# A one-core kernel in which each expert's TensorE program is set to a fixed place of its instruction blocks, with repeated waits left out

## What is computed

```python
def _moe2_ref(x, w_gate, w1, w2, capacity):      # 1536 tokens of 384, 8 experts, hidden 1024
    logits = x @ w_gate
    expert_idx = np.argmax(logits, axis=1)
    ...
    disp[e, counts[e]] = x[i]                    # each token into a row of its expert, at most 384 rows
    ...
    h = np.maximum(np.einsum('ecd,edf->ecf', disp, w1), 0.0)
    y = np.einsum('ecf,efd->ecd', h, w2)
    out[i] = gate_w[i] * y[expert_idx[i], pos[i]]
```

## Time and profile before

| | |
|---|---|
| runs: median, lowest, highest | 443.18, 442.60, 444.14 us |
| the profiled execution | 441.74 us, of which its span is 440.0 us |
| TensorE, matmuls | 413.5 us busy, 94% of the span |
| VectorE, ScalarE, GpSimd | 252.3, 192.7, 227.1 us busy |
| granted TensorE clock | 0.986 of full, mean of the span |

### The profile page before, as it was taken

How to read it: one execution, slowest core, us unless ns; L and a number is a source line. 1 busy time by engine, 2 the same in 40 slices (tenths; PEclk the granted TensorE clock), 3 DMA queues, 4 the chain that set the end, 5 groups by cost and what they waited for, 6 DMA issues and landing times.

```text
span 440.0 us, 9260 instructions
## 1 busy us (share of the span) xinstructions
PE 413.5 (94%) x3247; PEld 395.4 (90%) x3247; DVE 252.3 (57%) x515; ACT 192.7 (44%) x442; POOL 227.1 (52%) x237
## 2 busy tenths in 40 slices
PE   6799999999999999999999996889999999999783
PEld 5688889999999999999999995789999999998672
DVE  6888866766435434453347665353286696627840
ACT  2789944341311113111233332151668777437830
POOL 4999716554323533244365671521738476337942
PEclk9999999999999999999999999799999999999997
DMA  7996034536970100000003351285385786818300
GB/s 248 403 361 198 3 114 132 165 95 209 354 292 1 54 1 0 0 18 36 0 0 101 96 179 37 93 288 182 109 288 149 236 250 193 265 40 256 105 28 11
DMA packets 33938, 61.48 MB, mean 140 GB/s; under 512 B 4654, under 2 KB 26910, under 8 KB 33888
## 3 DMA queue, kind: packets, MB, share of 16 engines
q1 hardware_dynamic: 31008, 55.53, 38.4%
q0 software_dynamic: 2880, 5.29, 3.5%
HBM read 47.53 MB, written 14.79 MB: 142 GB/s over the span
## 4 chain that ended last, share of the span: by engine, by line
PE 79%; DVE 7%; ACT 5%; issue 4%; POOL 2%; DMA 0%; POOLq 0%; ACTq 0%; DVEq 0%
PE bank L1245 20%; PE bank L1260 20%; PE bank L1429 15%; PE bank L1393 10%; PE bank L1453 4%; ACT scores L632 3%; PE bank L1146 2%; PE bank L1360 1%; PE bank L1212 1%; ACT w_high L615 1%; DVE scores L879 1%; DVE neg L937 1%; PE bank L1176 1%; DVE act_full L943 1%; PE bank L1204 1%
## 5 line engine op out<-in xcount | busy, mean ns | idle before, releaser
L522 POOL TENSOR_TENSOR g_low<-act_full,g_high 128x384 fp32r<-128x384 f32 x63 | 63.6, 1010 | 114.6 <-ACT g_high L661 114.6
L661 ACT ACTIVATE g_high<-act_full 128x384 fp32r<-128x384 f32 x64 | 33.6, 526 | 149.9 <-DVE act_full L943 137.2
L1245 PE MATMUL bank<-x_split,w_high 128*128 (+1 forms) x384 | 98.4, 337 | 0.0
L937 DVE TENSOR_SCALAR neg<-bank,alpha_sb 128x384 f32<-128x384 f32 x64 | 39.2, 613 | 71.5 <-PE bank L1245 71.4
L589 POOL TENSOR_TENSOR w_low<-w_raw,w_high 128x384 fp32r<-128x384 f32 x48 | 50.0, 1074 | 46.9 <-ACT w_high L723 46.9
L1245 PEld LDWEIGHTS bank<-x_split,w_high 128*128 128x128 f32 x384 | 69.0, 188 | 0.2 <-issue 0.2
L1260 PE MATMUL bank<-w_high,g_high 128*128 128x384 f32 x189 | 65.1, 344 | 1.1 <-POOL g_low L522 1.1
L1245 PE MATMUL bank<-x_split,w_low 128*128 (+1 forms) x192 | 64.4, 336 | 0.0
L1260 PE MATMUL bank<-w_high,g_low 128*128 128x384 f32 x189 | 63.8, 337 | 0.0
L1260 PE MATMUL bank<-w_low,g_high 128*128 128x384 f32 x189 | 63.8, 337 | 0.0
L856 DVE TENSOR_TENSOR w_low<-w_raw,w_high 128x384 fp32r<-128x384 f32 x44 | 30.1, 689 | 28.5 <-ACT w_high L615 22.9
(11 more groups left out here) (138 smaller groups left out, 821.8 us busy)
## 6 DMA issues: line engine op xcount, KB each, us to landing
w_raw<-chunks SPq DMA_DIRECT2D x96, 192.0 KB, 4.5
w_raw<-chunks SPq DMA_DIRECT2D x32, 384.0 KB, 3.1
rk_in<-att_rk SPq DMA_DIRECT2D x12, 704.0 KB, 6.3
routed_rows<-fill SPq DMA_DIRECT2D x1, 5211.0 KB, 17.4
xe<-routed_rows SPq DMA_DIRECT2D x7, 579.0 KB
v_in<-att_v SPq DMA_DIRECT2D x12, 200.0 KB, 6.1
out<-fill SPq DMA_DIRECT2D x1, 2304.0 KB, 23.5
x_split<-x_split POOLq DMA_DIRECT2D x18, 48.0 KB, 2.5
```

The costliest lines, as they stand in the source:

```text
L522: pool.tensor_tensor(gl[:, f % 4, :], act_full[:, f % 2, :], gh[:, f % 4, :].bitcast(f32), ALU.subtract).then_inc(s_gl, 1)
L661: act.activation(gh[:, f % 4, :], act_full[:, f % 2, :], ACT.Copy).then_inc(s_gh, 1)
L937: dve.tensor_scalar(neg[:, f % 2, :], h, 0.0, alpha_sb[:, f:f + 1], ALU.min, ALU.mult)\
L1245: last = mm(bank[f % 4][:, 0:G], a[:, f, w], x[:, kc, bass.ds(g * G, G)], start=kc == 0 and i == 0, stop=kc == KC - 1 and i == 2)
```

## The change

It does two things to TensorE's program of the last stage, and nothing to the other engines.

Waits are left out where an equal or stronger one stands just before on the same engine. From expert 1 on, w_in's low parts are waited for at f = 0 and f = 4, four chunks at a time, not at each f; w_out's low parts once for all eight, at f = 0. The rows of experts 2 to 7 are waited for at their first tile alone, and the bank for tile 1's transposes with that for tile 0's. This makes experts 1 to 6 510 places long: 1, 78, 220, 1, 54 and 156.

```diff
@@ -52,6 +52,8 @@
     WARM = 3
     START_WARM = 22
     LEVELS = 7
+    FETCH = 256
+    INTO = 20
     RK = 4
     RH = 4
     assert P == 1 << LEVELS
@@ -1355,7 +1357,8 @@
                 if e == 1 and i == 0:
                     pe.wait_ge(s_tel, GT)
 
-                xe_there(pe, e, (i,))
+                if e < 2 or i == 0:
+                    xe_there(pe, e, (i,))
                 for kc in range(KC):
                     last = pe.transpose(dst[:, kc * P:(kc + 1) * P], xe[:, e % 2, i, kc * P:(kc + 1) * P], ident[:, :])
                 last.then_inc(s_te, 1)
@@ -1369,9 +1372,9 @@
 
             def x_bank_free(e, i):
 
-                if i < 2:
+                if i == 0:
                     y_bank_free(e, GT - 1 - i)
-                else:
+                elif i == 2:
                     pe.wait_ge(s_tel, e * GT + GT)
 
             def y_bank_free(e, i):
@@ -1381,7 +1384,10 @@
             def expert_up(e, f, n):
                 s = e * NFE + f
                 slot = s % SLOTS
-                w1_ready(pe, e, f)
+                if not e:
+                    w1_ready(pe, e, f)
+                elif f % HF == 0:
+                    w1_ready(pe, e, f + HF - 1)
                 if s >= 4:
 
                     pe.wait_ge(s_mgl, s - 3 + C_MGL)
@@ -1424,7 +1430,10 @@
                         pe.wait_ge(s_fl, 2 * e + f // HF + 1)
                     else:
                         pe.wait_ge(s_mgl, s + 1 + C_MGL)
-                    pe.wait_ge(s_wl2, s + NF + 1)
+                    if not e:
+                        pe.wait_ge(s_wl2, s + NF + 1)
+                    elif not f:
+                        pe.wait_ge(s_wl2, e * NFE + NFE + NF)
                     for m, (a, w) in enumerate(((egh, wh), (egh, wl), (egl, wh))):
                         last = mm(bank[4 + i][:, 0:DM], a[:, f, i * P:(i + 1) * P], w[:, s % SLOTS, W1:CW],
                                   start=f == 0 and m == 0, stop=f == NFE - 1 and m == 2)
@@ -1484,6 +1493,9 @@
                 turn_xe(0, i, bank[4 + i])
 
             for e in range(E):
+                if e:
+
+                    pe.addr_align(FETCH, offset=FETCH - INTO, max_nops=4)
                 with pe.If(rows[e] < P + 1):
                     pe.wait_ge(s_tel, e * GT + GT - 1)
                     pe.sem_inc(s_mh, NFE)
```

## The result

The changed kernel is slower: 447.18 us (445.14 to 449.64, 12 runs) against 442.87 us (441.95 to 444.14, 12 runs) of the kernel before beside it, a ratio of 1.0098 (95% interval 1.0078 to 1.0119). The forecast was 441.4 us with a range to 445.2. The profiled execution took 448.58 us, for a span of 446.8 us against 440.0. The twelve runs lie in two groups, six from 445.14 to 446.56 us and six from 447.79 to 449.64; the profiled one is of the upper group, so its 6.75 us more of span are more than the 4.31 us between the medians.

What follows compares the result with a forecast made beforehand. TensorE, busy 94% of the span, was taken to bound the kernel, with three instruction-fetch gaps near the end. Gains of 0.21 + 1.28 + 0.26 = 1.75 us, waits and padding 0, gave 443.18 - 1.75 = 441.4 us, range 439.8 to 445.2.

Steps and rivals of the forecast that it cites:

- What bounds the kernel: TensorE fills 94% of the span; three pieces of "issue" in the last three experts are instruction blocks arriving.
- The three gaps: TensorE pauses of 1.48, 1.28 and 0.26 us in the last three experts' tiles, read as waits for instructions.
- (a): Fixed places put each short branch's tile inside one block, removing its gaps: 0.21 + 1.28 + 0.26 = 1.75 us gained.
- second and third gaps: Pauses in the last two experts' tiles, claimed worth all of their 1.28 and 0.26 us.
- The first gap: Pause of 1.48 us in the third last expert's tile, claimed worth 0.21 us because VectorE's chain follows.
- cap in the scatters: Last scatter could start at 432.60; its forerunner at 431.06 allows 432.34, so scatters were taken not to limit the gain.
- The stated range: Range of 8 in 10 for the time, from 439.8 (3.02 plus 0.2 of the waits) to 445.2 us.
- both stretches are longer, if the packet starts promptly: Short experts have 4.9 and 6.2 us before needing the next block, against 2.3 to 2.8 us for its arrival.
- first rival: Blocks come late in a new place: three TensorE stands of 1.4 us at short experts' jumps, 445.0 us, chance 0.20.
- lies inside one block: The short branch's tile, offset 300 to 353, crosses no block boundary, so the three pauses cannot stay where they are.
- (c): Padding before experts, including some 220 dead places jumped before expert 1: 0 taken, bounds 0 to 1.5 us lost.
- (b): Leaving out repeated waits on TensorE: 0 taken, bounds 0 to 0.2 us gained.

Runs made afterwards that it cites:

- INTO = 120: Changed kernel with each expert from 1 on starting 120 places ahead of a block boundary, not 20: 440.61 us, ratio 0.9963; in more rounds 440.55 us, 0.996.
- added jump: Changed kernel plus one taken jump over one dead place, right behind the boundary at place 20, short branch only: 440.59 us, ratio 0.9967.
- control: Changed kernel plus the same dead place in the short branch, walked through as a filler instruction instead of jumped over: 447.15 us, ratio 1.0109.
- the last experiment: Kernel before with all its waits and one fixed place at expert 5, so experts 5 to 7 enter every block by a jump: 440.7 us, ratio 0.9965.

## Why the prediction was wrong, step by step

**What bounds the kernel: right.** The three gaps were the arrival of blocks, on the grid I had counted. The kernels with boundaries at 120, or with experts 5 to 7 moved, lose the second and the third. The other 27 of the 30 blocks before cost nothing that TensorE's chain shows. Expert 6's jump waited for its block: the branch of 415.77 lasts 3.37 us, where the taken ones of the kernel before last 0.21 to 0.37 us. The added jump and its control show that a jump can also set when the next block is asked for (packet at 410.76 with it, 416.61 without).

**(a), the worth of the gaps: right in size, where the blocks come in time.** TensorE's last matmul ends at 431.16 us with INTO = 120, against 432.86: 1.70 us earlier, forecast 1.75. That it comes so near is in part luck. Counted from expert 0's third tile (298.66 against 298.37) it is 1.99 us: 1.54 for the second and third gaps, nothing for the first, where I had 0.21, and most of the rest because a tile without a gap inside runs quicker (24 matmuls in 4.43 us in expert 7, 2.15 + 2.57 = 4.72 before). The first gap is worth next to nothing: INTO = 120 still has it (1.38 us), the added jump's kernel has not, and expert 6's tile starts at 416.07 and 416.88 in them, which is the same when counted from expert 0's third tile (298.66 and 299.48). Of the 1.70 us, though, only 1.23 reach the end. I had found no cap in the scatters; there is one, since the first of the last three waits for earlier ones to land. In the chain, and then the timeline of GpSimd, with INTO = 120:

```profile
425.11 4.27 DMA out<-y_out,token
...
425.11 0.97 POOL L580 DMA_INDIRECT out<-y_out,token  x1 [0.30 <-issue]
430.57 0.97 POOL L580 DMA_INDIRECT out<-y_out,token  x1 [4.49 <-issue]
431.84 0.97 POOL L580 DMA_INDIRECT out<-y_out,token  x1 [0.30 <-issue]
433.12 0.97 POOL L580 DMA_INDIRECT out<-y_out,token  x1 [0.30 <-issue]
```

The last starts at 433.12, not at the forecast 432.60, against 434.35 in the earlier trace rows; its forerunner, which I had left at 431.06, moved to 431.84.

The stated range has a slip that decides nothing: 443.18 less 3.02 and 0.2 is 439.96 us, not 439.8.

**The step that failed: "both stretches are longer, if the packet starts promptly".** I had 4.9 us from the boundary at 20 to the tile, against 2.3 to 2.8 us for a block, and took the request as made when the boundary is crossed. In expert 6 it was made only at the jump (415.77, packet 416.77), 4.17 us ahead of the first matmul. A row that warned of it stood in the prediction: the earlier trace rows, a packet 3.2 to 4.2 us late "with no other reason in sight". I gave it to the first rival with a chance of 0.20, and priced it there as a delay of that length, three times: 4.2 us less what is hidden. In fact expert 5 had no stand (its packet came 1.5 us after it walked in), expert 6 one of 3.67 us, expert 7 one of 1.08. The trace of before held, and I did not read, that all six packets of its last three experts start behind a taken jump; if only a jump asks, the 4.9 us are not there, and the stand is the whole of a fetch.

**That the branch's tile "lies inside one block": wrong for expert 7.** It has some 40 places fewer than the others (44 in the program before, less the left-out waits that stood among its missing transposes), which puts the start of its tile at about 260, and the tile over the boundary at 276. I had used the shorter program for the grid of before and forgot it here. That is its 1.08 us, after five matmuls, with the packet (432.46) again behind the jump (431.40).

**(c), padding at nothing: wrong, inside the bounds.** The jump over the 220 dead places lands 20 places ahead of a boundary, and the packet of the block behind it follows only then: jump 312.77, packet 313.88, the next jump (313.12), over that boundary, is held up for 3.17 us, and there are 0.78 us without matmuls ahead of 316.81. I took 0 and had a bound of 1.5. With 120 places ahead nothing is lost.

**The clock: left out of every case.** A stand of 3.67 us costs 1.95 us more after it, and expert 7's 19 matmuls took 4.91 us where 19/24 of 4.43 is 3.51: 1.40 us more. These 3.35 us are half of the profiled execution's 6.75, and more than the 2.2 us by which 445.0 for the late blocks fell short of the 447.18 measured.

**(b), the waits at nothing: right**, by the last experiment.

What stays open: why a walked boundary brings the next request after 1.5 us (expert 5 of the changed kernel) or 3.1 us (expert 7 of the control) at one place and not in 7.5 us or more at another (experts 6 and 7 of the changed kernel, 6 of the control); and why the gap of 1.08 us in expert 7's tile, 1.1 us of matmuls behind another of 0.61, let the clock fall, while 0.58 and then 1.28 us in the kernel before did not. It is open too why the packets behind the jumps of 402 to 403 us start late (3.65 to 3.98 us in the kernels with a jump there). The DMA engines are busy then (0.95 over 403 to 408 us in the changed kernel). But the added jump's packet of 410.76 came 1.5 us behind its jump with them at 0.80 to 1.00, so that alone does not explain it, and no run took the load away.

## What to carry to other kernels

Count where the instruction blocks' boundaries fall on the path that is taken, and ask of each what asks for the block behind it: a path should jump some 4 us of work before it needs a new block (3.3 to 4.5 us from jump to matmul here), and should not count on a boundary that it walks over to bring the block behind the next jump. Where the layout can't be changed, one jump over a dead place, early in the block, does as well (a ratio to the kernel before of 0.9967 where it was 1.0098). Price a stand of TensorE as long as those here (2.52 to 4.47 us) with the slow matmuls that follow (1.5 to 2.8 us more), and give a piece of "issue", or a wait whose releaser looks unlikely, to the instruction queue only after its packets have been laid beside it.

## What was not expected of the hardware

- In the last three experts most packets on q8 start 1.0 to 1.7 us behind a taken jump (0.65 to 2.05 us over all traces), and 3.65 to 3.98 us behind the jumps of 402 to 403 us. Of the short experts that walk over a boundary at their place 20, one in the changed kernel got its next packet 1.5 us later and two only by the jump 7.5 and 7.9 us on.
- Where TensorE wants a block that is not there, the first matmul comes 2.2 to 3.5 us after its packet starts: 434.70 - 432.46 = 2.24 and 419.94 - 416.77 = 3.17 us.
- The granted clock fell after each stand of 2.52 to 4.47 us, whether a block was missing or not (24 matmuls in 5.9 to 7.2 us for 4.4), and stayed full after 1.69, 1.46 and 1.33 us; once it fell after 1.08 us, behind another gap of 0.61.
- Of 70 long-met waits written in a row 33 instructions stand in the trace, most of them with two waits each, and each takes TensorE's sequencer 0.11 us.
